# Output projections as three products of high and low halves, with the split w_out held in buffers of the feed-forward part

## What is computed

```python
scores = q @ k.T / 8;  keep each row's 32 largest;  x = softmax(scores) @ v          # 4 x 8 heads, 576 x 576
gate = sigmoid(conv5(x));  val = x @ w_val;  y = (gate * val) @ w_out                 # 576 x 512 per batch
u = y + real(fft(fft(y, tokens), features))
un = (u - mean(u)) / sqrt(var(u) + 1e-6)
out = u + relu(un @ w_ch1) @ w_ch2                                                    # 512 -> 2048 -> 512
```

## Time and profile before

| | us |
|---|---|
| three runs: lowest, median, highest | 1085.76, 1088.55, 1089.21 |
| the profiled execution: its time | 1087.9 |
| the profiled execution: its span | 1085.7 |
| PE busy, share of the span | 994.5, 92% |
| VectorE busy | 830.2, 76% |
| ScalarE busy | 624.0, 57% |
| GpSimd busy | 333.7, 31% |

### The profile page before, as it was taken

One profiled execution on the slowest core, in us unless ns is written; L12 is line 12 of the kernel. 1 busy time (PEld: TensorE's weight loads), 2 busy tenths in 40 slices (PEclk: granted clock), 3 DMA queues, 4 the chain that ended last, 5 costly groups with the idle time before them and its releaser, 6 DMA issues.

```text
span 1085.7 us, 19701 instructions
## 1 busy us (share of the span) xinstructions
PE 994.5 (92%) x6848; PEld 779.3 (72%) x6848; DVE 830.2 (76%) x1804; ACT 624.0 (57%) x1349; POOL 333.7 (31%) x474
## 2 busy tenths in 40 slices
PE   5876777899999999999999999999999999999997
PEld 3454555676688887766777888766778887668896
DVE  7999999898999997969988877889998953120000
ACT  5888678555676766546666665556666662122211
POOL 2575353022332222123322213133322222243221
PEclk9987768899999999999999999999999999999999
DMA  7466546112267776212667464321466674239874
GB/s 224 158 196 197 175 166 228 53 40 70 100 212 264 251 280 224 85 29 57 240 212 274 160 224 172 104 62 50 173 228 232 248 259 155 78 117 359 298 247 131
DMA packets 78113, 190.91 MB, mean 176 GB/s; under 512 B 9408, under 2 KB 27584, under 8 KB 78016
## 3 DMA queue, kind: packets, MB, share of 16 engines
q1 hardware_dynamic: 77872, 189.41, 50.9%
q10 hardware_dynamic: 144, 0.26, 0.1%
HBM read 168.14 MB, written 21.50 MB: 175 GB/s over the span
## 4 chain that ended last, share of the span: by engine, by line
PE 74%; DVE 12%; ACT 7%; issue 5%; DMA 0%; POOL 0%; ACTq 0%; DVEq 0%; POOLq 0%
PE p_m L707 17%; PE p_m L722 17%; PE p_m L581 12%; PE p_t L570 8%; PE p_t L554 7%; DVE rest L926 6%; PE p_s L541 5%; DVE top L932 4%; PE p_m L611 3%; ACT prob L799 2%; ACT pT L813 2%; PE p_m L601 2%; PE p_t L574 1%; DVE top L917 1%; PE p_m L646 1%
## 5 line engine op out<-in xcount | busy, mean ns | idle before, releaser
L932 DVE MAX8 top<-rest 128x8 f32<-128x576 f32 x432 | 304.3, 745 | 0.0
L926 DVE MATCH_REPLACE8 rest<-top,rest 128x576 f32<-128x576 f32 x288 | 211.5, 741 | 0.0
L1140 POOL TENSOR_TENSOR hid_lo<-hid,hid_hi 128x256 fp32r<-128x256 f32 (+1 forms) x128 | 104.8, 818 | 339.4 <-ACT hid_hi L872 339.2
L722 PE MATMUL p_m<-w_st,hid_hi 128*128 128x512 f32 x576 | 182.7, 398 | 0.4 <-POOL hid_lo L1140 0.4
L707 PE MATMUL p_m<-un_hi,w_st 128*128 128x256 f32 (+1 forms) x1024 | 165.3, 304 | 13.5 <-ACT hid_hi L872 13.5
L788 ACT ACTIVATE s_all<-p_s 128x576 f32<-128x576 f32 x143 | 92.5, 647 | 122.3 <-PE p_s L541 103.3
L707 PEld LDWEIGHTS p_m<-un_hi,w_st 128*128 128x128 f32 x1024 | 142.3, 189 | 26.3 <-issue 23.5
L554 PE MATMUL p_t<-id_sb,prob 128*128 128x128 f32 x720 | 117.0, 295 | 34.9 <-ACT prob L805 34.5
L871 ACT ACTIVATE hid<-p_m 128x256 f32<-128x256 f32 (+1 forms) x128 | 51.3, 400 | 137.4 <-PE p_m L707 137.3
L570 PE MATMUL p_t<-pT,v_sb 128*64 128x128 f32 (+1 forms) x1600 | 110.1, 289 | 17.3 <-ACT pT L813 17.3
L554 PEld LDWEIGHTS p_t<-id_sb,prob 128*128 128x128 f32 x720 | 82.1, 147 | 60.1 <-ACT prob L805 40.2
(11 more groups left out here) (107 smaller groups left out, 1481.8 us busy)
## 6 DMA issues: line engine op xcount, KB each, us to landing
w_st<-w_split SPq DMA_DIRECT2D x256, 512.0 KB, 4.5
w_split<-w_st SPq DMA_DIRECT2D x32, 512.0 KB, 3.0
u<-w_ch SPq DMA_DIRECT2D x32, 256.0 KB, 3.8
k_raw<-kT SPq DMA_DIRECT2D x16, 288.0 KB, 3.2
v_sb<-v SPq DMA_DIRECT2D x16, 256.0 KB, 3.5
wslot<-w_val SPq DMA_DIRECT2D x4, 1024.0 KB, 5.3
wslot<-w_out SPq DMA_DIRECT2D x4, 1024.0 KB, 5.2
out<-u SPq DMA_DIRECT2D x16, 256.0 KB, 2.5
```

The source lines that it names most:

```text
L722: mm = pe.matmul(mbank(j), h[i % 2][:, P * j:P * j + P], w2_st[i % NB2][:, w, :], start=f == 0 and part == 0, stop=f == FC - 1 and part == 2)
L926: dve.match_replace(rest[tt % 2][:, :], top[tt % NK][:, 8 * n - 8:8 * n], src, LOWEST).then_inc(s_chain, 1)
L932: found = dve.max(top[tt % NK][:, 8 * n:8 * n + 8], rest[tt % 2][:, :])
L1140: pool.tensor_tensor(hid_lo[i % 2][:, 0:width(b, g)], hid[:, 0:width(b, g)], hid_hi[i % 2][:, 0:width(b, g)].bitcast(F32), ALU.subtract).t ...
```

## The change

`project` no longer multiplies float32 `gv` by float32 `w_out`. It adds three products of float32r halves: high by high, high by the weight's low, low by high. Its parts:

- `high_gv` (ScalarE) and `low_gv` (GpSimd) make the halves of `gv` in the three `zed` steps, in the tensors `un_hi` and `un_lo`, which the feed-forward part of the batch before no longer needs.
- w_out is split once, as 4 more parts (32 to 35) of the same pipeline, into HBM (`wout_split`). Of its 4 blocks of 128 features, block 0 stays in a new tensor `w_out0`; for each batch, block 1 is loaded into the fourth buffer of w_ch1, block 2 into the third of w_ch2, and block 3 in four pieces of 256 columns into `hid_hi` and `hid_lo`.
- `wslot` keeps w_val for the whole run; its reloads are gone. `load_w1` and `load_w2` for the two borrowed buffers wait until all projections of the batch are done (m_y).
- `z_last` now lies in `hid`.
- `hidden` alternates between banks 2 and 3 where `hidden_bank` says so, and waits only for the relu of the step that last used its bank.

```diff
@@ -92,8 +92,20 @@
-HIDDEN_BANK = [2, 3]
+def hidden_bank(b, g, f):
+    if g == 0:
+        return 3 if f == 1 or f >= 12 and f % 2 == 0 else 2
+    return 2 if b % 2 == 0 and f % 2 else 3
+def hidden_before(i):
+    place = [hidden_bank(j // FC // 2, j // FC % 2, j % FC) for j in range(i + 1)]
+    return max((j for j in range(i) if place[j] == place[i]), default=None)
@@ -124,6 +136,8 @@
+PARTS = 2 * FC + KC
@@ -180,8 +194,10 @@
+        wout_split = nc.dram_tensor("wout_split", (KC, P, 2, DM), F32).ap()
+        w_out0 = sb("w_out0", [P, 2, DM], F32R)
...
@@ -224,10 +239,14 @@
+        z_last = hid[:, 0:NCOS]
+        gv_hi, gv_lo = un_hi, un_lo
...
@@ -380,6 +401,25 @@
         def folded(c, o, m):
+        def out_rows(b, r):
+            return slice(0, LEFT) if r == NR - 1 and b % 2 == 0 else slice(0, P)
+        def gv_cols(b, r):
+            return slice(ROWS[r][0], ROWS[r][0] + out_rows(b, r).stop)
+        def w_out_part(b, k):
+            if k == 0:
+                return w_out0[:, :, :]
+            if k == 1:
+                return w1_st[(2 * FC * b + NB1 - 1) % NB1][:, :, :, :].rearrange("p h k n -> p h (k n)")
+            return w2_st[(2 * FC * b + NB2 - 1) % NB2][:, :, :]
+        def w_out_last(h, half):
+            return (hid_lo if h else hid_hi)[half][:, 0:DM // 2]
@@ -428,7 +468,9 @@
-                    if i < FC:
+                    if i >= 2 * FC:
+                        sp.dma_start(w_raw[i % NRAW][:, :], w_out[P * f:P * f + P, :]).then_inc(s_wraw[i % NRAW], 16)
+                    elif i < FC:
@@ -437,28 +479,41 @@
                 def keep_part(i):
-                    if i < FC:
+                    if i >= 2 * FC:
+                        n = i - FC
+                        sp.dma_start(wout_split[f], w2_st[n % NB2][:, :, :].bitcast(F32)).then_inc(s_w2put[n % NB2], 16)
+                    elif i < FC:
                 def load_w1(i):
+                    if i % (2 * FC) == NB1 - 1:
+                        sp.wait_ge(m_y, NR * (i // (2 * FC) + 1))
                 def load_w2(i):
+                    if i % (2 * FC) == NB2 - 1:
+                        sp.wait_ge(m_y, NR * (i // (2 * FC) + 1))
                 def step(what, b, n):
-                    if (what, n) == ("val", 2 * KC - 1):
-                        sp.wait_ge(m_val, 2 * KC * (b + 1))
-                        sp.dma_start(wslot[:, :, :], w_out.rearrange("(c q) n -> q c n", q=P)).then_inc(m_wout, 16)
-                    elif (what, n) == ("ch0", 1) and b < B - 1:
-                        sp.wait_ge(m_y, NR * (b + 1))
-                        sp.dma_start(wslot[:, :, :], w_val.rearrange("(c q) n -> q c n", q=P)).then_inc(m_wval, 16)
+                    if (what, n) == ("val", 0):
+                        if b:
+                            sp.wait_ge(m_h, 2 * FC * b)
+                            sp.wait_ge(m_acc, 2 * FC * b)
+                        for k in (1, 2):
+                            sp.dma_start(w_out_part(b, k).bitcast(F32), wout_split[k]).then_inc(m_wout, 16)
+                        for h in range(2):
+                            for half in range(2):
+                                c0 = DM // 2 * half
+                                sp.dma_start(w_out_last(h, half).bitcast(F32),
+                                             wout_split[KC - 1, :, h, c0:c0 + DM // 2]).then_inc(m_wout, 16)
@@ -498,14 +553,16 @@
-                        if i + NRAW < 2 * FC:
+                        if i + NRAW < PARTS:
+                    if i == PARTS - 1:
-                            sp.wait_ge(s_w2put[j], 16 * ((FC - 1 - j) // NB2 + 1))
+                            sp.wait_ge(s_w2put[j], 16 * ((PARTS - FC - 1 - j) // NB2 + 1))
+                        sp.dma_start(w_out0[:, :, :].bitcast(F32), wout_split[0]).then_inc(m_wout, 16)
@@ -623,7 +680,8 @@
                 def values(b, j):
-                        pe.wait_ge(m_wval, 16 * (b + 1))
+                        if b == 0:
+                            pe.wait_ge(m_wval, 16)
@@ -668,15 +726,25 @@
                 def project(b, r):
-                        pe.wait_ge(m_wout, 16 * (b + 1))
+                        pe.wait_ge(m_wout, 16 + 96 * (b + 1))
+                        pe.wait_ge(m_gvlo, (KC + 1) * (b + 1))
-                    mm = chain(mbank(PROJ_BANK[r]), rows(b, r), 0, DM, [gv_rows(k, r) for k in range(KC)],
-                               [wslot[:, k, :] for k in range(KC)])
+                    bank = mbank(PROJ_BANK[r])[out_rows(b, r), :]
+                    for n, (x, h) in enumerate(((gv_hi, 0), (gv_hi, 1), (gv_lo, 0))):
+                        for k in range(KC):
+                            if k < KC - 1:
+                                pieces = [(0, DM, w_out_part(b, k)[:, h, :])]
+                            else:
+                                pieces = [(0, DM // 2, w_out_last(h, 0)), (DM // 2, DM, w_out_last(h, 1))]
+                            for c0, c1, w in pieces:
+                                mm = pe.matmul(bank[:, c0:c1], x[:, k, gv_cols(b, r)], w, start=n + k == 0,
+                                               stop=n == 2 and k == KC - 1, skip_group_check=True)
@@ -688,6 +756,7 @@
+                        pe.wait_ge(m_hev, 2 * FC * b + 2)
@@ -699,12 +768,14 @@
-                    if i:
-                        pe.wait_ge(m_hev, i)
+                    if hidden_before(i) is not None:
+                        pe.wait_ge(m_hev, hidden_before(i) + 1)
+                    if g == 0 and f == 12:
+                        pe.wait_ge(m_unT, 2 * NR * (b + 1))
-                            mm = pe.matmul(mbank(HIDDEN_BANK[g], n), w1_st[i % NB1][:, w, k, :], x[:, k, at:at + n],
+                            mm = pe.matmul(mbank(hidden_bank(b, g, f), n), w1_st[i % NB1][:, w, k, :], x[:, k, at:at + n],
...
@@ -841,6 +913,13 @@
+                def high_gv(b, n):
+                    if n == 2:
+                        act.activation(gv_hi[:, :, un_cols(b, NR - 1)], gv[:, :, 0:GV_LO], ACT.Copy).then_inc(m_gvhi, 1)
+                    for c in {2: (0,), 0: (1, 2), 1: (3,)}[n]:
+                        act.activation(gv_hi[:, c, 0:2 * HALF], gv[:, c, GV_LO:S], ACT.Copy).then_inc(m_gvhi, 1)
@@ -848,6 +927,7 @@
+                        high_gv(b, n)
...
@@ -1098,6 +1178,18 @@
+                def low_gv(b, n):
+                    done = (KC + 1) * b
+                    if n == 2:
+                        pool.wait_ge(m_gvhi, done + 1)
+                        cols = un_cols(b, NR - 1)
+                        pool.tensor_tensor(gv_lo[:, :, cols], gv[:, :, 0:GV_LO], gv_hi[:, :, cols].bitcast(F32),
+                                           ALU.subtract).then_inc(m_gvlo, 1)
+                    for c in {2: (0,), 0: (1, 2), 1: (3,)}[n]:
+                        pool.wait_ge(m_gvhi, done + 2 + c)
+                        pool.tensor_tensor(gv_lo[:, c, 0:2 * HALF], gv[:, c, GV_LO:S], gv_hi[:, c, 0:2 * HALF].bitcast(F32),
+                                           ALU.subtract).then_inc(m_gvlo, 1)
...
```

More of the change, by code:

```diff
@@ L218, in build @@
         z = sb("z", [P, 2, DM])
-        z_last = sb("z_last", [P, NCOS])
         ab = sb("ab", [P, DM])
@@ L282, in build @@
         m_zev = sem("m_zev")
+        m_gvhi = sem("m_gvhi")
+        m_gvlo = sem("m_gvlo")
         m_ab = sem("m_ab")
@@ L351, in part_due @@
         def part_due(s, lag=0):
-            return s - lag - SPLIT_AT if 0 <= s - lag - SPLIT_AT < 2 * FC else None
+            return s - lag - SPLIT_AT if 0 <= s - lag - SPLIT_AT < PARTS else None
         def conv_due(s):
@@ L828, in split_weights @@
                         act.wait_ge(s_w1put[f % NB1], 16 * (f // NB1))
-                    if i >= FC and f >= NB2:
-                        act.wait_ge(s_w2put[f % NB2], 16 * (f // NB2))
+                    n = i - FC
+                    if n >= NB2:
+                        act.wait_ge(s_w2put[n % NB2], 16 * (n // NB2))
                     act.activation(part_tile(i)[:, 0, :], w_raw[i % NRAW][:, :], ACT.Copy).then_inc(s_whi, 1)
@@ L869, in step @@
                         act.wait_ge(m_h, i + 1)
-                        bank = mbank(HIDDEN_BANK[g], width(b, g))
+                        bank = mbank(hidden_bank(b, g, n), width(b, g))
                         act.activation(hid[:, 0:width(b, g)], bank, ACT.Relu).then_inc(m_hf, 1)
@@ L1123, in step @@
                         fold_tokens(b, n // 2)
+                    elif what == "zed":
+                        low_gv(b, n)
                     elif what == "seq":
```

## The result

| | before | after |
|---|---|---|
| median of the runs on one chip (us) | 1087.15 (1084.31 to 1089.21, 4 runs) | 1075.37 (1073.19 to 1077.64, 4 runs) |
| profiled execution: time, span (us) | 1087.9, 1085.7 | 1073.24, 1071.2 |

A forecast was written before the change was run, and what follows sets the result against it. PE was taken to bound the projections and everything after 880 us, with VectorE near its limit behind batches 0 and 2's projections. Terms -13.0 - 3.4 - 1.2 - 0.3 + 0.3 + 1.9 = -15.7 us; forecast 1072.5 us, range 1067 to 1081.

The forecast's parts named there:

- 13.0 us for the projections: All 20 projections: each falls from 3.43 to 2.78 us on PE, saving 0.65 us, together 13.0 us.
- 4.9 for the banks: Feed-forward `hidden` steps: fewer waits for the relu, saving 3.4 us, 1.2 at step 1 of batches 0 and 2, 0.3 last batch.
- the bound I had named below (2.76): Lower bound for one projection, with its six products of 256 columns at 0.115 us each: 2.76 us.
- 0.8 us to spare: Last batch, before the first projection: the last half is ready about 938.2, PE arrives 938.99, so no wait.
- the 1.4 us that I left on `sums` 0 of batches 0 and 2: Step 1's relu wait of 1.98 us moves to `sums` 0, where 1.4 us stays; gain 0.6 us per batch.
- the 0.6 in the last batch: Last batch: of step 1's wait of 0.90 us, 0.6 stays before `sums` 0, which needs `hid_lo`; gain 0.3 us.
- 1.98 + 0.8 for GpSimd's subtraction - 1.42: Wait left before `sums` 0 in batches 0 and 2: old wait plus subtraction, less one `hidden`, giving 1.4 us.
- the `un` wait of 0.3 us in the last batch: Second transpose, last batch: PE arrives 2.6 us earlier, `un` only 2.0, adding 0.3 us of wait.
- +1.9 for what attention takes back in exponents and score copies: Batches 0 to 2: step-1 gains of 1.2 us lost to exponent waits, plus ScalarE copies delaying score copies; together 1.9 us.
- Rival A: VectorE takes back half of what PE gains beside attention; 1077.5 us, chance 0.17.
- Rival B: Late loads into the borrowed weight buffers starve the last feed-forward, PE waiting 2.9 us; 1075.4 us, chance 0.05.
- Rivals C and D: C: gains beside attention vanish, 1084.6 us, chance 0.05. D: ScalarE's copies in `zed` slots delay selection, 1092.8 us, chance 0.03.

The follow-up runs named there:

- e_dev: The kernel after, with the fifth `deviation` moved behind the subtraction of `hidden` 1 in GpSimd's queue; 1066.32 us, ratio to before 0.9818.
- e_banks: The kernel before with only the new banks of `hidden`, projections still float32; 1079.09 us, ratio to before 0.9925.
- e_banks_cost: The kernel before with the new banks and the planner's price of a projection at 2.8 instead of 3.5; 1075.75 us, ratio to before 0.9899.
- e_halves: The kernel before with the halves of `gv` made and waited for, but read by nothing; 1085.84 us, ratio to before 0.9998.
- e_cost: The kernel after with only the planner's price of a projection changed, 2.8 instead of 3.5; 1066.62 us, ratio to before 0.9809.

## Why the prediction was right, and where not

- **Right in sum, wrong in shares.** PE bounds the kernel, and both parts gain. But I had 13.0 us for the projections and 4.9 for the banks; alone they gave 5.4 and 8.2. Most of what PE saves in the projections is given back in waits right behind them, and the errors below nearly cancel, which is luck.
- **Mis-sized: -13.0 for 20 projections.** A projection takes 2.87 us, not 2.78: 2.76 once PE is in float32r products (9 x 0.23 + 6 x 0.115), and 0.1 to 0.2 more where it follows float32 work. That is the bound I had named below (2.76) plus a start that no row of before showed for a float32r product behind a float32 one. 20 x 0.57 = 11.3 us.
- **Right: the halves cost nothing and the first projection does not wait.** I had 0.8 us to spare. The last subtraction in after starts at 924.92 and takes 1.27, so it ends at 926.19, and PE comes at 926.88: 0.7. The parts of w_out were not split near 205 to 235 us but earlier (the last subtraction starts at 194.38); no wait hangs on it.
- **Wrong: the 1.4 us that I left on `sums` 0 of batches 0 and 2, and the 0.6 in the last batch.** They are 2.09, 2.09 and 0.92, and batch 1 has 1.93 where I had none. The step that failed is "1.98 + 0.8 for GpSimd's subtraction - 1.42": it counts the subtraction from the relu's copy alone, and not what stands ahead of it in GpSimd's queue. The fifth `deviation` waits there for VectorE; moving it halved the wait (e_dev). Shorter projections make it worse, since PE comes earlier and the chain behind the fifth projection does not: 3.9 us in e_banks, 8.2 in after.
- **Wrong place: the `un` wait of 0.3 us in the last batch.** There it is 0.21. But the same coupling costs 1.42 and 1.47 us in batches 0 and 2, beside attention, where I had not looked for it because `un` was always early in the trace of before. I had worked it out from the distance of projections in the last batch, where the sum of the third block follows its projection by 0.3 us; beside attention it stands behind the selection and follows by 3.7.
- **Wrong: +1.9 for what attention takes back in exponents and score copies.** Exponent waits fell by 1.1 us and VectorE kept its slack but for 0.6 us. What attention takes back shows in the two waits above instead, as far as the selection holds up the sums. The sum of the terms as measured: -11.3 for projections, +2.3 for relu, `hid_lo` and `un` together (forecast -4.6), -1.1 for exponents, which is -10.1 against a net of -12.4; the remaining 2.3 lie in gaps I did not trace.
- **Rival A** gave 1077.5, 2.1 us from the median where the forecast is 2.9 off. Its own signs (exponent or `gv` waits up by 4 us) are absent: 5.0 us for `gv` as before. Two waits on the chain behind the projections, 9.0 us of them in batches 0 to 2, took much of the gain there. But VectorE is a link of that chain, and beside attention its selection stands ahead of the sums; so the rival is refuted in its signs, not in its engine.
- **Rival B** is not seen in after. The price of a late load does exist: 1.9 us once, in e_banks_cost, which has no borrowed buffers at all. **Rivals C and D** fell with the times and with e_halves.

## What to carry over

A step that gets shorter brings its successor forward, so cost the successor's inputs by their whole queue: the instruction that makes an input may stand behind one that waits for a third engine. Where a plan lays steps by a table of prices, run the change under more than one price: with 2.8 instead of 3.5 the same 20 projections were worth 9.8 us instead of 3.7, and the kernel before, with no projection shorter, gained 4.8. And take the size of an edit from a run with that edit alone before tuning around it.

## What the runs showed of the hardware

- **The clock behind short waits.** In the stretches above PE runs at 2.4 GHz nearly throughout, and falls to 1.2 for 3.4 us or a multiple in or shortly behind PE's longer waits: before at 462.8 (0.6 us behind the end of the wait of 3.38 us for `gv`) and 770.0 (1.4 behind one of 1.98), after at 457.4 (0.8 behind one of 3.38) and 761.2 (1.0 behind one of 2.09). The two products at 286.78 in e_cost take 1.22 us, and 0.73 at 951.71 in after. So a wait can cost more than itself, and taking one away can give more: e_dev has lost the drop at 761.2, where its wait is 1.29 us, and e_banks the one at 770.0, where its wait is 1.25. Why 2.09 us at 760.15 in after go with a drop and 2.09 us at 288.29 in the same run do not, these runs do not tell.
- **The first float32r product behind float32 work** of 512 columns takes 0.42 us to the next start instead of 0.23 (926.88 in after), and 0.34 in the fifth projection (944.91).
- **The first fifth of the run varies by itself.** The start of the same transposes of `prob`, in PE's timeline; between before and after only four parts of weights more are split ahead of it, and between after and e_dev nothing differs there:

before

```profile
202.58 0.76 PE L554 MATMUL p_t<-id_sb,prob 128*128 128x128 f32 x5 [1.91 <-ACT prob L805]
```

in after

```profile
200.50 0.76 PE L611 MATMUL p_t<-id_sb,prob 128*128 128x128 f32 x5 [1.91 <-ACT prob L876]
```

and in e_dev

```profile
197.35 0.81 PE L611 MATMUL p_t<-id_sb,prob 128*128 128x128 f32 x5 [1.92 <-ACT prob L876]
```

Over the fourteen profiled executions it lies between 197.35 and 202.83 us. A few us between two kernels' medians are therefore laid to an edit only where the net differences and the waits say the same (as the 3.7 and 9.8 us above). The cause stays open.
